# A fused attention, gated-MLP and convolution kernel: three summed attention terms for the second slot group, low parts of w_v on VectorE, a softmax split in five, and new instruction orders

## The chip, the cores and the metric

The kernel runs on one core of a Trainium2 chip. Its time is the device time in microseconds of one execution; lower is better. The time before is the median of three timed executions. The profile is of one further execution, so its own time stands beside its span.

## The reference

x is (2, 4160, 192), all data fp32. Three stages follow one another:

```python
# 1: attention over 7 taps, 8 heads of 24 channels; the weights are a softmax over the taps
w = softmax(weight_gen, axis=-1)                 # (2, 4160, 8, 7)
x = einsum('bshk,bskhg->bshg', w, unfold(x))     # row s sees rows s-6 .. s
# 2: channel mix with 1024 hidden columns
xk = mu_k * x + (1 - mu_k) * x_prev;  xr = mu_r * x + (1 - mu_r) * x_prev
k = relu(xk @ w_k);  v = (k * k) @ w_v;  y = sigmoid(xr @ w_r) * v
# 3: 1024 hidden columns, a convolution over 3 rows as a gate
h = relu(y @ w_in);  c = sum(conv_w[k] * h shifted by k - 1);  out = (h * sigmoid(c)) @ w_out
```

## The kernel before, in words

The 8320 rows of x are laid out as 128 partitions of 65 consecutive rows ("slots"). Slots are worked in 17 groups, `SIZES = [2, 4, ..., 4, 3]`; group g passes through attention, stage 2 and stage 3. The convolution of stage 3 works on window w, the same slots moved back by one, one group later. The hidden 1024 columns are 8 chunks c of 128.

Nothing is scheduled on the fly: each engine has a written order of calls (`first_steps`, then `step(i)` in a loop, then `last_steps`), and semaphores keep data right. An instruction whose data isn't there holds everything behind it on its engine. The calls that matter:

- Softmax: `softmax_front(g)` on VectorE (max, subtract), `exps(g)` on ScalarE, `softmax_back(g)` on VectorE (sum, reciprocal, product), in place in `wgt`. `SM_ENDS` splits the 66 rows of weights; a part is named by the first group that needs it: 0, 3, 7 and 11.
- Attention: `att_mult(g, k)` and `att_add(g, k)` on VectorE, 7 products and up to 6 sums. For a group in `TERMS` the taps are summed in several terms, and TensorE adds the terms up: `term_part` and the last `t_part` multiply each with the identity into PSUM (`mid`). For other groups `t_part` only transposes. `double` and `double_term` on ScalarE copy 64 channels beside themselves, for the second part.
- Mix: `z_part` (ScalarE, from PSUM), `mix_k`, `mix_r`, `mix_2` (VectorE). `x_hi`, `xr_hi_part` (ScalarE) and `x_lo`, `xr_lo_part` (VectorE) split each value into a rounded part and the rest, since fp32r products are used on TensorE: five products (`up_products`) stand for one fp32 product.
- Stage 2: `up1(g, c)`, then `k_relu`, `k_square`, `k_cast` (ScalarE), `k_lo` (VectorE), `down1(g, c)`; `r_part`, `r_sigmoid`; at the end `y_mult`, `y_hi_part`, `y_lo_part`.
- Stage 3: `up2(g, c)`, `h_relu`, `first_tap` (ScalarE), `conv_before`, `conv_after` (VectorE), `gate_sigmoid` (ScalarE), `gate` (VectorE), `down2(w, c)`, `o_copy`, and `carry`, which keeps the last slots of h.
- Weights: each is split into a rounded part and a low part. For w_k and w_v TensorE makes the low part: `low_wk`, `low_wv` add the raw weights times the identity and the rounded ones times minus the identity, `keep_wk`, `keep_wv` (ScalarE) copy it out. For w_r and w_in VectorE subtracts (`split_wr`, `split_wi`).
- `warm(n)` issues n transposes whose result nobody reads.

ScalarE uses the tables of exp and of sigmoid; each change between them is an ACT_TABLE_LOAD. DMAs of the start are issued by SP and, for the parameter rows, w_r and the first rows of the weights, by ScalarE.

The diff touches nearly every line of the written orders and these functions: the table `TERMS` (line 193), `low_wv` (408), `down1` (496), `exps` (1167), `load_wr` (1190), `keep_wv` (1207), `vals` (2238), `softmax_front` (2250), `softmax_back` (2262) and SP's list of loads (295 to 317).

Of the kernel before, what the change touches and what calls it, by code (L numbers as in the profile page):

```python
# [5 lines left out]
F32 = mybir.dt.float32  # L6
F32R = mybir.dt.float32r
ALU = mybir.AluOpType
# [6 lines left out]
def mixer_kernel(nc, x, weight_gen, mu_k, mu_r, w_k, w_v, w_r, w_in, conv_w, w_out, out):  # L15
# [58 lines left out]
    with ctx:  # L74
# [99 lines left out]
        SM_ENDS = [0, FIRST[3] + 1, FIRST[7] + 1, FIRST[11] + 1, TPP + 1]  # L174
# [18 lines left out]
        TERMS = {0: ((0, 1), (2, 3), (4,), (5, 6))}  # L193
# [89 lines left out]
        def _(sp):  # L283
# [9 lines left out]

            S0 = size(0)
# [8 lines left out]
            for n, arrived in ((1, wg2_in), (2, wg3_in)):  # L303
                lo, hi = SM_ENDS[n], SM_ENDS[n + 1] if n == 1 else TPP + 1
                sp.dma_start(wgt[:, lo * WROW:hi * WROW], wg_rows[:, (lo - 1) * WROW:(hi - 1) * WROW])\
                  .then_inc(arrived, 16)
# [5 lines left out]
            for g in range(UNIFORM + 1, 6):  # L312
                load_x(g)
            for w in range(1, NG):
                store(w)
                if w + 5 < NG:
                    load_x(w + 5)
# [27 lines left out]
        def _(pe):  # L345
# [62 lines left out]
            def low_wv(k):  # L408
                pair = slice(2 * k, 2 * k + 2)
                if k == 0:  # L410

                    pe.wait_ge(prm_ok, 1)
                if k >= 1:
                    pe.wait_ge(wv_split, 2 * k)
                low_part(od[0][:, 0:2 * D].rearrange("p (c n) -> p c n", c=2), raw_wv[:, pair, :],
                         wv_parts[:, pair, 0:D], (wv_in, 16), wv_cast, k // 2 + 1, lowv_done)

# [124 lines left out]
            def first_steps():  # L542
                term_part(0, 0, 1)
                term_part(0, 2, 1)
                term_part(0, 0, 2)
                term_part(0, 1, 1)
                term_part(0, 2, 2)
                t_part(0, 1)
                term_part(0, 1, 2)
                t_part(0, 2)  # L550
                low_wk(0)
                low_wk(1)
                low_wv(0)
# [4 lines left out]
                low_wv(1)  # L558
                up1(0, 2)
                up1(0, 3)  # L560
                r_part(0, 1)
                r_part(0, 2)
                up1(0, 4)
                warm(3)
                down1(0, 0)
                up1(0, 5)
                down1(0, 1)
                low_wv(2)
                down1(0, 2)
                t_part(1, 1)  # L570
                down1(0, 3)
                up1(0, 6)
                up1(0, 7)
                t_part(1, 2)
                low_wv(3)
# [4 lines left out]
                warm(11)  # L580
# [7 lines left out]
                r_part(1, 1)  # L588
                up2(0, 7)
                up1(1, 0)  # L590
                r_part(1, 2)
                up1(1, 1)
                up1(1, 2)
                up1(1, 3)
                up1(1, 4)
                down1(1, 0)
                up1(1, 5)
                down1(1, 1)
                up1(1, 6)
                t_part(2, 1)  # L600
                down1(1, 2)
                up1(1, 7)
                down1(1, 3)
                down1(1, 4)
                down1(1, 5)
                t_part(2, 2)
# [9 lines left out]
                up2(1, 6)  # L616
                up2(1, 7)
                r_part(2, 1)
                up1(2, 0)
                up1(2, 1)  # L620
                r_part(2, 2)
                up1(2, 2)
                down2(1, 0)
                down2(1, 1)
                up1(2, 3)
                up1(2, 4)
                down2(1, 2)
                down1(2, 0)
                up1(2, 5)
                down1(2, 1)  # L630
                up1(2, 6)
                down1(2, 2)
                up1(2, 7)
                down1(2, 3)
                down1(2, 4)
                t_part(3, 1)
                down1(2, 5)
                down1(2, 6)
                down1(2, 7)
                t_part(3, 2)  # L640
                down2(1, 3)
                down2(1, 4)
                up2(2, 0)
                up2(2, 1)
                up2(2, 2)
                up2(2, 3)
                down2(1, 5)
                up2(2, 4)
                up2(2, 5)
                down2(1, 6)  # L650
                up2(2, 6)
                up2(2, 7)
                r_part(3, 1)
                up1(3, 0)
                up1(3, 1)
                r_part(3, 2)
# [5 lines left out]
                up1(3, 5)  # L662
                down1(3, 1)
                up1(3, 6)
                down1(3, 2)
                up1(3, 7)
                down1(3, 3)
                down1(3, 4)
                down2(2, 0)
                t_part(4, 1)  # L670
                down1(3, 5)
                down1(3, 6)
                down1(3, 7)
                t_part(4, 2)
                down2(2, 1)
                down2(2, 2)
                up2(3, 0)
                up2(3, 1)
                up2(3, 2)

            def step(i):
                down2(i - 2, 3)
                up2(i - 1, 3)
                up2(i - 1, 4)
                up2(i - 1, 5)
                down2(i - 2, 4)
                up2(i - 1, 6)
                up2(i - 1, 7)
                down2(i - 2, 5)
                down2(i - 2, 6)  # L690
                r_part(i, 1)
                up1(i, 0)
                up1(i, 1)
                r_part(i, 2)
                up1(i, 2)
                down2(i - 2, 7)
                up1(i, 3)
                up1(i, 4)
                down1(i, 0)
                up1(i, 5)  # L700
                down1(i, 1)
                up1(i, 6)
                down1(i, 2)
                up1(i, 7)
                down1(i, 3)
                down1(i, 4)
                down2(i - 1, 0)
                t_part(i + 1, 1)
                down1(i, 5)
                down1(i, 6)  # L710
                down1(i, 7)
                t_part(i + 1, 2)
                down2(i - 1, 1)
                down2(i - 1, 2)
                up2(i, 0)
                up2(i, 1)
                up2(i, 2)

            def last_steps():
                down2(NG - 8, 3)  # L720
                up2(NG - 7, 3)
                up2(NG - 7, 4)
                up2(NG - 7, 5)
                down2(NG - 8, 4)
                up2(NG - 7, 6)
                up2(NG - 7, 7)
                down2(NG - 8, 5)
                down2(NG - 8, 6)
                r_part(NG - 6, 1)
                up1(NG - 6, 0)  # L730
                up1(NG - 6, 1)
                r_part(NG - 6, 2)
                up1(NG - 6, 2)
                down2(NG - 8, 7)
                up1(NG - 6, 3)
                up1(NG - 6, 4)
                down1(NG - 6, 0)
                up1(NG - 6, 5)
                down1(NG - 6, 1)
                up1(NG - 6, 6)  # L740
                down1(NG - 6, 2)
                up1(NG - 6, 7)
                down1(NG - 6, 3)
                down1(NG - 6, 4)
                down2(NG - 7, 0)
                t_part(NG - 5, 1)
                down1(NG - 6, 5)
# [2208 lines left out]
```

## Time and profile before

| | us |
|---|---|
| median of three timed executions | 717.82 |
| lowest, highest | 717.74, 718.28 |
| the profiled execution | 718.39 |
| its span, first to last instruction | 716.6 |
| TensorE busy | 706.2 (99%) |
| VectorE busy | 668.5 (93%) |
| ScalarE busy | 634.9 (89%) |
| granted TensorE clock | 1.00 over the span |

PE is TensorE, DVE VectorE, ACT ScalarE, SP SyncE; PEld is TensorE's weight load. Times are microseconds from the first instruction of the span. A matmul's duration is longer than the step from one to the next, because they overlap in the array; likewise VectorE's and ScalarE's instructions overlap their neighbours by about 0.1 us. Of a stall, the row names the engine or DMA whose event came last.

### The profile page before, as it was taken

How to read it: one execution, taken by the hardware profiler on the slowest of the kernel's cores; microseconds unless marked ns; L12 is line 12 of the kernel's file. 1: busy time of each engine (PE TensorE's matmuls, PEld its weight loads, DVE VectorE, ACT ScalarE, POOL GpSimd, SP SyncE). 2: the span in 40 equal slices, each digit the busy share in tenths (PEclk: the TensorE clock that was granted, in tenths of full speed). 3: DMA queues.
4: the chain of work that ended last, by engine and by line, in shares of the span. 5: the costliest groups of instructions: out<-in, count | busy, mean ns of one | idle time of the engine just before them, and what ended most of it. 6: DMA issues, size and time to landing. Idle time of an engine off the chain costs nothing.

```text
span 716.6 us, 10616 instructions
## 1 busy us (share of the span) xinstructions
PE 706.2 (99%) x3537; PEld 601.3 (84%) x3537; DVE 668.5 (93%) x982; ACT 634.9 (89%) x1280; POOL 3.6 (0%) x12
## 2 busy tenths in 40 slices
PE   7999999999999999999999999999999999999998
PEld 7777788888888888888887888888888888888998
DVE  6999999999999999999999999999999999987686
ACT  4998998999989899897999989998998989898975
POOL 1000000000000000000000000000000000000000
PEclk9999999999999999999999999999999999999999
DMA  9502010200202020020200102020110202000001
GB/s 257 189 27 96 1 55 1 55 23 2 78 1 77 1 77 1 1 79 0 78 1 14 65 1 78 1 78 1 26 53 1 77 1 73 1 22 1 24 1 49
DMA packets 10107, 29.86 MB, mean 42 GB/s; under 512 B 1326, under 2 KB 4936, under 8 KB 9926
## 3 DMA queue, kind: packets, MB, share of 16 engines
q1 hardware_dynamic: 9244, 28.89, 12.4%
q8 instruction: 28, 0.46, 0.3%
q10 hardware_dynamic: 810, 0.30, 0.2%
q14 instruction: 25, 0.20, 0.1%
HBM read 21.75 MB, written 6.39 MB: 39 GB/s over the span
## 4 chain that ended last, share of the span: by engine, by line
PE 81%; DVE 14%; issue 3%; ACT 2%; POOL 0%; DVEq 0%; POOLq 0%; ACTq 0%
PE up L424 34%; PE od L537 19%; PE dn L509 4%; PE dn L493 4%; PE dn L516 4%; PE dn L513 4%; PE dn L512 4%; PE dn L515 3%; DVE att L2103 2%; DVE prod L2085 2%; DVE gat L2236 2%; DVE cv L2208 2%; PE od L964 2%; PE mid L348 2%; DVE cv L2221 1%
## 5 line engine op out<-in xcount | busy, mean ns | idle before, releaser
L537 PE MATMUL od<-wo_sb,gat 128*128 128x192 f32 x1024 | 181.7, 326 | 0.1
L537 PEld LDWEIGHTS od<-wo_sb,gat 128*128 128x128 f32 x1024 | 169.9, 190 | 6.4 <-ACT o_sb L1111 0.4
L2167 DVE TENSOR_TENSOR kq_lo<-ksq,kq_hi 128x512 fp32r<-128x512 f32 (+2 forms) x136 | 90.3, 666 | 15.1 <-ACT kq_hi L1053 14.1
L1082 ACT ACTIVATE cv<-h,prm 128x512 f32<-128x512 f32 x128 | 91.7, 716 | 10.9 <-DVE gat L2236 10.3
L2208 DVE SCALAR_TENSOR_TENSOR cv<-h,prm,cv 128x512 f32<-128x512 f32 x128 | 94.9, 749 | 3.5 <-ACT cv L1082 2.4
L2221 DVE SCALAR_TENSOR_TENSOR cv<-h,prm,cv 128x512 f32<-128x512 f32 x128 | 95.6, 749 | 0.6
L2236 DVE TENSOR_TENSOR gat<-h,cv 128x512 f32<-128x512 f32 (+1 forms) x136 | 89.0, 664 | 5.2 <-ACT cv L1100 3.4
L2085 DVE TENSOR_TENSOR prod<-xin,wgt 128x768 f32<-128x768 f32 (+1 forms) x100 | 93.3, 934 | 0.0
L2103 DVE TENSOR_TENSOR att<-att,prod 128x768 f32<-128x768 f32 (+1 forms) x97 | 91.2, 941 | 0.1
L1074 ACT ACTIVATE h<-up 128x512 f32<-128x512 f32 (+2 forms) x136 | 77.4, 570 | 13.9 <-PE up L424 13.8
L1100 ACT ACTIVATE cv<-cv 128x512 f32<-128x512 f32 (+1 forms) x136 | 81.6, 605 | 5.1 <-DVE cv L2221 4.4
L1037 ACT ACTIVATE ksq<-up 128x512 f32<-128x512 f32 (+2 forms) x136 | 78.1, 579 | 7.5 <-PE up L424 4.7
L1053 ACT ACTIVATE kq_hi<-ksq 128x512 fp32r<-128x512 f32 (+2 forms) x136 | 81.7, 614 | 2.9 <-PE dn L516 1.0
L1044 ACT ACTIVATE ksq<-ksq 128x512 f32<-128x512 f32 (+2 forms) x136 | 81.6, 613 | 0.7
L424 PE MATMUL up<-y_hi,wi_hi 128*128 128x512 f32 (+2 forms) x136 | 59.2, 435 | 0.2 <-ACT h L1074 0.2
L509 PE MATMUL dn<-kq_hi,wv_parts 128*128 128x512 f32 (+2 forms) x136 | 55.3, 406 | 1.0 <-DVE kq_lo L2167 0.6
L424 PE MATMUL up<-xk_hi,wk_hi 128*128 128x512 f32 (+2 forms) x136 | 55.1, 405 | 1.0 <-ACT ksq L1037 0.9
L424 PE MATMUL up<-xk_s,wk_hi 128*128 128x512 f32 (+2 forms) x136 | 52.2, 384 | 1.2 <-DVE xk_s L2147 1.2
L424 PE MATMUL up<-y_lo,wi_hi 128*128 128x512 f32 (+2 forms) x136 | 52.5, 386 | 0.2 <-DVE y_lo L2187 0.2
L424 PE MATMUL up<-y_t,wi_lo 128*128 128x512 f32 (+2 forms) x136 | 52.6, 387 | 0.1
L424 PE MATMUL up<-y_hi,wi_lo 128*128 128x512 f32 (+2 forms) x136 | 52.4, 385 | 0.0
L516 PE MATMUL dn<-kq_lo,wv_parts 128*128 128x512 f32 (+2 forms) x136 | 52.3, 385 | 0.0
(137 smaller groups left out, 1362.2 us busy)
## 6 DMA issues: line engine op xcount, KB each, us to landing
xin<-in_x SPq DMA_DIRECT2D x14, 960.0 KB, 4.8
out<-o_sb SPq DMA_DIRECT2D x16, 384.0 KB, 3.9
wgt<-in_weight_gen SPq DMA_DIRECT2D x1, 1092.0 KB, 14.2
h<-h SPq DMA_DIRECT2D x1, 1024.0 KB, 4.5
xin<-in_x SPq DMA_DIRECT2D x1, 864.0 KB, 4.4
h<-in_moe_w_v SPq DMA_DIRECT2D x1, 768.0 KB, 10.2
wo_sb<-in_moe_w_out SPq DMA_DIRECT2D x1, 768.0 KB, 15.7
h<-in_moe_w_k SPq DMA_DIRECT2D x1, 512.0 KB, 7.1
```

What stands on the lines that cost most here:

```text
L424: mm = nc.tensor.matmul(dst[:, 0:n], w[:, cols], a[:, 0:n], start=(t == 0), stop=(t == len(terms) - 1))
L509: nc.tensor.matmul(dn[0][:, 0:n], w[:, 0:P], k_hi, start=(c == 0), stop=False)
L537: mm = nc.tensor.matmul(o, tile[:, b * P:(b + 1) * P], wo_sb[:, c, :], start=(c == 0 and b % 2 == 0), stop=(c == NC - 1), skip_group_check ...
L1044: nc.scalar.activation(ring(ksq, c, n), ring(ksq, c, n), ACT.Square).then_inc(ksq_ok, 1)
L1053: nc.scalar.activation(ring(kq_hi, c, n), ring(ksq, c, n), ACT.Copy).then_inc(kqh_ok, 1)
L1082: nc.scalar.activation(conv_tile(w, c), win(w, c, 0), ACT.Copy, scale=prm[:, 3 + NC + c:4 + NC + c])\
L2085: nc.vector.tensor_tensor(v, x, w, ALU.mult).then_inc(x_used if k == TAPS - 1 else at_mul, 1)
L2103: nc.vector.tensor_tensor(acc, acc, v, ALU.add)\
L2167: nc.vector.tensor_tensor(ring(kq_lo, c, n), ring(ksq, c, n), ring(kq_hi, c, n).bitcast(F32), ALU.subtract).then_inc(kql_ok, 1)
L2208: nc.vector.scalar_tensor_tensor(o, win(w, c, -1), prm[:, 3 + c:4 + c], base, ALU.mult, ALU.add)\
L2221: nc.vector.scalar_tensor_tensor(o, win(w, c, 1), prm[:, at:at + 1], o, ALU.mult, ALU.add)\
L2236: nc.vector.tensor_tensor(gate_tile(w, c), win(w, c, 0), conv_tile(w, c), ALU.mult).then_inc(g_ok, 1)
```

## The change

Five things are done, and the orders of all engines are written anew around them.

1. Group 1 joins `TERMS` with three terms, (0, 1), (2, 3) and (4, 5, 6): VectorE does four adds for it, not six; TensorE does four `term_part`, and its `t_part` are sums with the identity. ScalarE does `double_term(1, 0)` and `(1, 1)`.
2. The low parts of w_v are two subtractions on VectorE (`split_wv`); `low_wv` on TensorE and `keep_wv` on ScalarE are gone.
3. `SM_ENDS` has a further end: parts of 3, 8, 16, 16 and 23 rows, the second one named by group 1. `exps(0)` is followed by the copy to `minus`; the one-column sigmoid `early`, which loads the table of sigmoid, follows `exps(1)`.
4. SP loads the parameter rows and w_r; ScalarE's queue loads the two halo runs of x of the second batch. The last two loads of weight_gen become one.
5. `load_x` is issued one group later than before, the loops run to NG - 5, and `warm` calls are placed anew: after the parameter rows' transpose 1 instead of 28, then 23, 6, 4, 2, 8 and 16 instead of 3, 11 and 16.

```diff
-        SM_ENDS = [0, FIRST[3] + 1, FIRST[7] + 1, FIRST[11] + 1, TPP + 1]
+        SM_ENDS = [0, FIRST[1] + 1, FIRST[3] + 1, FIRST[7] + 1, FIRST[11] + 1, TPP + 1]
...
-        TERMS = {0: ((0, 1), (2, 3), (4,), (5, 6))}
+        TERMS = {0: ((0, 1), (2, 3), (4,), (5, 6)), 1: ((0, 1), (2, 3), (4, 5, 6))}
...
-            for a, b in HALO_RUNS:
+            for a, b in HALO_RUNS[:2]:
                 sp.dma_start(xin[a:b, 0:TAPS * D], before(x_flat, a, b, TAPS, D)).then_inc(x_in, 16)
+            for r, src in enumerate((mu_k, mu_r)):
+                sp.dma_start(prm_rows[r:r + 1, :], src[0:P].rearrange("(a n) -> a n", a=1)).then_inc(prm_in, 16)
+                sp.dma_start(prm_rows[2:3, r * D2:(r + 1) * D2], src[P:D].rearrange("(a n) -> a n", a=1))\
+                  .then_inc(prm_in, 16)
+            sp.dma_start(prm_rows[3:NPRM, :], conv_w.rearrange("k (c p) -> (k c) p", p=P)).then_inc(prm_in, 16)
+            load_wgt(SM_ENDS[1], SM_ENDS[2], wg2_in)
             load_up_weights(sp, w_k, 0, wk_in)
+            for c0, c1, at in ((0, D, 0), (P, D, D)):
+                sp.dma_start(raw_wr[:, 0, at:at + c1 - c0], w_r[0:P, c0:c1]).then_inc(wr_in, 16)
+                sp.dma_start(raw_wr[0:D2, 1, at:at + c1 - c0], w_r[P:D, c0:c1]).then_inc(wr_in, 16)
+                sp.dma_start(raw_wr[D2:P, 1, at:at + c1 - c0], w_r[P:D, c0:c1]).then_inc(wr_in, 16)
             sp.dma_start(xin[:, (TAPS + S0) * D:XSLOTS * D], x_rows[:, S0 * D:EDGE * D]).then_inc(x2_in, 16)
             sp.dma_start(raw_wv, w_v.rearrange("(c p) n -> p c n", p=P)).then_inc(wv_in, 16)
             load_up_weights(sp, w_in, 2, wi_in)
...
+            load_wgt(SM_ENDS[2], TPP + 1, wg3_in)
...
-                if eq(g, 0) and c % 2 == 0:
-                    pe.wait_ge(wv_split, c + 2)
+                if eq(g, 0) and c == 0:
+                    pe.wait_ge(wv_split, 2)
...
                 if eq(g, 0):
+                    act.wait_ge(id_ok, 2)
+                    nc.scalar.activation(minus[:, :], ident[:, :], ACT.Copy, scale=-1.0).then_inc(minus_ok, 1)
+                if eq(g, 1):
 
                     act.wait_ge(id_ok, 2)
                     nc.scalar.activation(early[:, :], ident[:, 0:1], ACT.Sigmoid).then_inc(early_ok, 1)
-                    load_wr()
-                    nc.scalar.activation(minus[:, :], ident[:, :], ACT.Copy, scale=-1.0).then_inc(minus_ok, 1)
...
+            for a, b in HALO_RUNS[2:]:
+                act.dma_start(xin[a:b, 0:TAPS * D], before(x_flat, a, b, TAPS, D)).then_inc(x_in, 16)
...
+            def split_wv():
+                dve.wait_ge(wv_cast, 2)
+                nc.vector.tensor_tensor(wv_parts[:, :, 2 * P:3 * P], raw_wv[:, :, 0:P],
+                                        wv_parts[:, :, 0:P].bitcast(F32), ALU.subtract).then_inc(wv_split, 1)
+                nc.vector.tensor_tensor(wv_parts[:, :, D:2 * P], raw_wv[:, :, P:D],
+                                        wv_parts[:, :, P:D].bitcast(F32), ALU.subtract).then_inc(wv_split, 1)
```

ScalarE's order of the start, new (one line stands for the calls in this order):

```
exps(0); double_term(0,1), (0,2), (0,0); exps(1); cast_wk(); double(0); z_part(0,0), (0,1); cast_wr(); x_hi(0,1);
z_part(0,2); xr_hi_part(0,1); keep_wk(0), (1); x_hi(0,2); keep_wk(2); xr_hi_part(0,2); z_carry(0); cast_wi(0); ...
```

VectorE's order of the start, new:

```
softmax_front(0); softmax_back(0); att_mult(0,0), (0,1); att_add(0,1); att_mult(0,2), (0,3), (0,4); att_add(0,3);
softmax_front(1); att_mult(0,5), (0,6); params(); att_add(0,6); softmax_back(1); mix_k(0); mix_r(0); att_mult(1,0);
x_lo(0,1); mix_2(0); att_mult(1,1); x_lo(0,2); att_add(1,1); split_wr(); xr_lo_part(0,1); att_mult(1,2), (1,3);
xr_lo_part(0,2); att_add(1,3); att_mult(1,4), (1,5); k_lo(0,0); att_mult(1,6); split_wv(); att_add(1,5); k_lo(0,1);
att_add(1,6); k_lo(0,2), (0,3); split_wi(0); k_lo(0,4); split_wi(1); mix_r(1); mix_k(1); k_lo(0,5), (0,6);
att_mult(2,0); k_lo(0,7); att_mult(2,1); y_mult(0,1), (0,2); y_lo_part(0,1), (0,2); mix_2(1); x_lo(1,1); ...
```

TensorE's order of a steady step, new. Before, `down2(w, 0)` to `(w, 2)` stood between `down1(g, 4)` and `up2(g, 0)`, the other five among up2 and the next up1:

```
up1(g,5); down2(w,0); down1(g,1), (g,2); up1(g,6); down1(g,3); up1(g,7); down1(g,4); down2(w,1); t_part(g+1,1);
down2(w,2); t_part(g+1,2); down1(g,5) .. (g,7); down2(w,3) .. (w,5); up2(g,0) .. (g,7); r_part(g+1,1), (g+1,2);
up1(g+1,0) .. (g+1,2); down2(w,6); up1(g+1,3); down2(w,7); up1(g+1,4); down1(g+1,0)         with w = g - 1
```

The later softmax parts on VectorE. Before: front(7) after `k_lo(1,5)`, back(7) after `att_mult(5,3)`; front(11) after `conv_before(7,1)`, back(11) after `conv_after(8,3)`. New: front(7) after `gate(3,1)` and back(7) after `gate(4,4)`; front(11) after `gate(7,1)`, back(11) after `gate(8,4)`, which in both cases is followed by one more gate, mix_r and y_mult. `exps(3)` on ScalarE stood after `h_relu(0,6)` and stands after `k_cast(1,3)`.

## Rows read from the trace of the kernel before

**Rows 1.** From the page: busy time by engine; the chain that ended last, by engine.

```profile
PE 706.2 (99%) x3537; PEld 601.3 (84%) x3537; DVE 668.5 (93%) x982; ACT 634.9 (89%) x1280; POOL 3.6 (0%) x12
...
PE 81%; DVE 14%; issue 3%; ACT 2%; POOL 0%; DVEq 0%; POOLq 0%; ACTq 0%
```

**Rows 2.** Busy by stretch: stretch, length, busy (instructions) per engine, clock, DMA share, GB/s.

```profile
231.19:272.67 41.48, 41.48 (x205) 35.26 (x203) 39.31 (x57) 37.17 (x74) 0.00 (x0) 1.00 0.10 34
...
314.15:399.61 85.46, 84.39 (x406) 69.87 (x406) 84.89 (x119) 77.69 (x151) 0.00 (x0) 1.00 0.11 33
```

**Rows 3.** The chain in order of time: start, us, engine, tile, line, count.

```profile
4.05 6.40 PE od L964 x30
...
13.83 4.04 PE mid L355 x36
...
51.50 1.28 ACT L1063
...
71.37 1.75 PE od L964 x16
...
141.89 1.30 PE od L537 x8
...
183.78 1.30 PE od L537 x8
...
225.53 1.30 PE od L537 x8
...
325.92 1.42 DVE smx L2259
327.36 1.50 DVE wgt L2260
...
378.29 1.42 DVE smx L2270
...
381.35 1.50 DVE wgt L2273
```

**Rows 4.** Timeline of VectorE, the start: start, us, line, operation, shapes, [idle before <- releaser].

```profile
4.24 0.80 DVE L2259 TENSOR_REDUCE smx<-wgt 128x88 f32<-128x616 f32 x1 [3.34 <-DMA wgt<-in_weight_gen]
...
9.37 0.76 DVE L2085 TENSOR_TENSOR gat<-xin,wgt 128x576 f32<-128x576 f32 x1
...
15.51 0.76 DVE L2103 TENSOR_TENSOR att<-att,prod 128x576 f32<-128x576 f32 x1
...
19.04 0.48 DVE L2135 SCALAR_TENSOR_TENSOR xr<-mid,prm,zr 128x256 f32<-128x256 f32 x1 [1.81 <-ACT zr L988]
```

**Rows 5.** Timeline of VectorE at y_mult(0,1) and x_lo(1,1).

```profile
41.56 0.43 DVE L2177 TENSOR_TENSOR y<-dn,y 128x256 f32<-128x256 f32 x1
...
42.24 0.68 DVE L2144 TENSOR_TENSOR xk_lo<-xk,xk_hi 128x512 fp32r<-128x512 f32 x1
```

**Rows 6.** Timeline of SP: the four loads of x's halo rows.

```profile
1.64 1.77 SPq L298 DMA_DIRECT2D xin<-in_x  x4
```

**Rows 7.** DMA issues: count, KB each, median us from issue to landing.

```profile
xin<-in_x SPq DMA_DIRECT2D x2, 252.0 KB, 5.2
```

**Rows 8.** Timeline of ScalarE in the start.

```profile
6.64 1.28 ACT L1178 ACT_TABLE_LOAD   x1
...
7.93 0.20 ACT L1178 ACTIVATE early<-ident 128x1 f32<-128x1 f32 x1
...
14.72 1.04 ACT L1199 ACTIVATE wk_hi<-h 128x1024 fp32r<-128x1024 f32 x1
...
18.43 0.57 ACT L988 ACTIVATE zr<-mid,omu 128x384 f32<-128x384 f32 x1
```

**Rows 9.** Timeline of TensorE around low_wv(1).

```profile
26.83 0.81 PE L398 MATMUL od<-h,ident 128*128 128x384 f32 x2
...
27.65 0.28 PE L424 MATMUL up<-xk_hi,wk_hi 128*128 128x256 f32 x1
```

**Rows 10.** Timeline of VectorE at y_mult(1,1).

```profile
71.48 0.69 DVE L2177 TENSOR_TENSOR y<-dn,y 128x512 f32<-128x512 f32 x1 [0.66 <-PE dn L516]
```

More of the change, by code:

```diff
@@ L969, in _ @@
             nc.tensor.transpose(od[0][:, 0:NPRM], prm_rows[:, :], ident[0:NPRM, 0:NPRM]).then_inc(prm_t, 1)
-            warm(28)
+            warm(1)
             first_steps()
-            for i in range(4, NG - 6):
+            for i in range(4, NG - 5):
                 step(i)
@@ L1381, in first_steps @@
+                k_square(2, 1)
+                k_relu(2, 2)
+                k_cast(2, 1)
+                r_sigmoid(2, 2)
+                k_relu(2, 3)
+                k_square(2, 2)
+                k_cast(2, 2)
+                k_square(2, 3)
+                gate_sigmoid(1, 2)
+                k_cast(2, 3)
+                k_relu(2, 4)
+                k_relu(2, 5)
+                k_square(2, 4)
+                gate_sigmoid(1, 3)
                 k_cast(2, 4)
                 k_square(2, 5)
+                first_tap(1, 5)
@@ L1499, in first_steps @@
+                k_relu(4, 1)
+                k_cast(4, 0)
+                k_square(4, 1)
                 gate_sigmoid(3, 2)
+                k_relu(4, 2)
+                k_cast(4, 1)
+                r_sigmoid(4, 2)
+                k_relu(4, 3)
+                k_square(4, 2)
+                o_copy(2, 0)
+                o_copy(2, 1)
+                k_cast(4, 2)
+                k_square(4, 3)
                 exps(7)
-                first_tap(3, 4)
-                r_sigmoid(4, 1)
+                k_cast(4, 3)
@@ new lines, in step @@
+                k_square(i + 1, 5)
+                first_tap(i, 6)
+                k_cast(i + 1, 5)
+                k_relu(i + 1, 6)
+                first_tap(i, 7)
+                k_square(i + 1, 6)
+                carry(i, 1)
+                k_cast(i + 1, 6)
+                k_relu(i + 1, 7)
+                double(i + 2)
+                k_square(i + 1, 7)
+                gate_sigmoid(i, 4)
+                k_cast(i + 1, 7)
+                gate_sigmoid(i, 5)
+                carry(i, 2)
@@ L1741, in last_steps @@
-                z_carry(NG - 4)
-                k_square(NG - 4, 3)
-                k_relu(NG - 4, 4)
+                k_relu(NG - 4, 2)
+                k_cast(NG - 4, 1)
+                r_sigmoid(NG - 4, 2)
+                k_relu(NG - 4, 3)
+                k_square(NG - 4, 2)
+                o_copy(NG - 6, 0)
+                o_copy(NG - 6, 1)
+                k_cast(NG - 4, 2)
+                k_square(NG - 4, 3)
+                k_cast(NG - 4, 3)
+                k_relu(NG - 4, 4)
+                k_relu(NG - 4, 5)
@@ L1888, in last_steps @@
+                k_cast(NG - 2, 1)
+                r_sigmoid(NG - 2, 2)
+                k_relu(NG - 2, 3)
+                k_square(NG - 2, 2)
+                o_copy(NG - 4, 0)
+                o_copy(NG - 4, 1)
+                k_cast(NG - 2, 2)
+                k_square(NG - 2, 3)
+                k_cast(NG - 2, 3)
+                k_relu(NG - 2, 4)
+                k_relu(NG - 2, 5)
+                first_tap(NG - 3, 5)
+                double(NG - 1)
+                k_square(NG - 2, 4)
                 gate_sigmoid(NG - 3, 3)
-                o_copy(NG - 4, 0)
@@ L2032, in _ @@
             first_steps()
-            for i in range(4, NG - 6):
+            for i in range(4, NG - 5):
                 step(i)
@@ L2755, in last_steps @@
             def last_steps():
+                x_lo(NG - 3, 2)
+                gate(NG - 4, 0)
+                att_add(NG - 2, 2)
+                conv_after(NG - 4, 1)
+                att_mult(NG - 2, 3)
+                conv_after(NG - 4, 2)
+                conv_before(NG - 4, 3)
+                att_mult(NG - 2, 4)
+                att_add(NG - 2, 3)
+                k_lo(NG - 3, 0)
+                gate(NG - 4, 1)
+                conv_after(NG - 4, 3)
                 conv_before(NG - 4, 4)
+                att_mult(NG - 2, 5)
@@ L2929, in _ @@
             first_steps()
-            for i in range(4, NG - 6):
+            for i in range(4, NG - 5):
                 step(i)
```

1916 lines of the change are left out of this document (829 added, 1087 removed).

## The prediction

> **What bounds the kernel now.** I read the page first: TensorE is busy 99% of the span and carries 81% of the chain that ended last, VectorE 14% [rows 1]. So I look for the places where TensorE does something other than needed work. The second view, busy time by stretch, answers for the middle. One group of four slots takes 41.48 us with TensorE busy in all of it and VectorE in 39.31; the stretch from 314.15 to 399.61 us holds two groups and takes 85.46 us instead of 82.96 [rows 2]. 2.5 us are lost there, and VectorE, busy 84.89 of 85.46, has no slack in it. In the chain in order of time one and the same down2 piece stands at 141.89, 183.78 and 225.53 us: periods of 41.89 and 41.75, 0.4 and 0.3 over. The 2.5 us lie around the softmax of the last 23 rows (front at 325.92, back at 378.29) [rows 3], the 0.7 us around the back part of the 16 rows before them. The third view, the timeline, is for the start: the first term part runs on TensorE at 13.83 [rows 3]; VectorE starts attention of slot group 0 at 9.37, its last add at 15.51, then waits 1.81 us for zr and mixes at 19.04 [rows 4]. From there to y_mult of group 0 at 41.56 [rows 5] it is nearly solid. So up to about 41 us VectorE sets the pace, with warm transposes on TensorE; after that TensorE does.
>
> **Part by part.**
>
> *First softmax part of 3 rows, not 11.* VectorE's passes fall from 616 to 168 elements. A pass of 616 took 0.80 us [rows 4], one of 1288 took 1.50 [rows 3]: 1.04 ns an element, so 168 cost 0.35. Reduce, subtract, exp, reduce, add, reciprocal and product come to some 2.5 us instead of the 5.1 from 4.24 to 9.33: ready at 6.7. Now the halo rows of x bind. Their last load was issued at about 3.0 [rows 6] and the larger ones land in 5.2 [rows 7], so at 8.2; with 224 KB less in front (0.9 us at the page's 257 GB/s) at 7.4, bounds 6.6 and 9.4. Attention of group 0 starts 1.9 us sooner.
>
> That lead is handed back before it reaches anything. Its nine steps are 0.68 each (from 9.37 to 15.51). Between them stands front(1), eight rows, 1.3 us, and params, 0.3: the last add begins at 7.4 + 6.1 + 1.6 = 15.1 against 15.51. On ScalarE exps(1) can't start before front(1) ends, 7.4 + 7 x 0.68 + 1.3 = 13.5. Behind it are queued exp 0.6, the load of the sigmoid table 1.29 and `early` 0.2, two casts of w_k of 0.95, double(0) 0.25 and two z parts of 0.5 [rows 8], a step being 0.1 less than a duration. The sum puts zr at 18.8 and the first mix at 18.9 against 19.04. The table load was hidden before (at 6.64, beside the softmax); its cover is gone. TensorE's own queue allows little more: 30 transposes end at 10.45 [rows 3], then a term of 0.67 (4.04 for six of them), warm(23) at 0.11 and four terms: t_part(0,1) at 16.5, so z at 17.4 at the earliest.
>
> The Trainium skill, page "ScalarE: Activation LUTs", section "What ACT_TABLE_LOAD costs", has a switch of tables cost the 1.28 us load and a drain of 1.38 more. Here the load at 6.64 is followed by the next activation at 7.93: 1.29 us and no drain [rows 8], and the measurement decides. By the page's 2.66 the start would come 1.4 us later and the whole change be worth 0.6 instead of 2.0.
>
> *From the mix to y_mult(0), on VectorE.* Added: split_wr, 0.7, which lay in the wait for zr before; split_wv, two passes of 1024 and 512 elements, 1.21 and 0.68 by the pass of 512 (0.68, [rows 5]) and 1.04 ns an element, as steps 1.74 (bounds 1.5 and 2.0). Gone: two att_adds of group 1, 768 elements, 0.87 each, 1.74. Net +0.7, less 0.1 for the earlier mix: y_mult(0) at about 42.1, 0.5 later. But x_lo(1,1), at 42.24 between y_mult and y_lo [rows 5], moves behind y_lo, and up2(0,0) needs y_lo in its third product: 0.5 comes back. I take 0 for up2(0,1), at 44.0; bounds -1.2 (table load hidden, x at 6.6) and +1.5 (x at 9.4, or ScalarE slips).
>
> *TensorE in the start.* low_wv goes: 26.83 to 27.65 is 0.82 [rows 9], four are 3.3 us. Term parts of group 1 are 4 x 8 matmuls at 0.112 (4.04 over 36, [rows 3]), 3.6 us; t_part(1) becomes 16 of them for 8 transposes, +0.9. Net +1.2 us, hidden by the waits for xr_lo, split_wv (down1(0,0) at 32.4 by the sum above) and k_lo; uncovered it costs 1.2. ScalarE loses the eight copies of keep_wv (about 2.1 us as steps) and gains two doubles (0.6). SP issues five parameter loads and six of w_r ahead of x2, w_v and w_in; the bytes in front of w_in are what they were, so it lands where it did. load_x(w + 4) now stands behind store(w), which waits for the copy of the last down2 of window w; its x is used some 20 us later by the order of the steps and takes 5 to land, so nothing. The parameters, now behind halo rows in one queue, must be there when the transposes end at 10.45; I expect 7.5 to 8.5, so nothing is paid.
>
> *Group 1.* exps(3) brings two table loads; the chain runs through the one at 51.50 [rows 3], in front of r_sigmoid and k_relu. In the new order it stands behind k_cast(1,3), with no sigmoid until the gates; front(7), 2 us of VectorE, leaves the stretch before y_mult(1). The warm(16) at 71.37 stays [rows 3]. I take -0.5, bounds -1.1 and +0.5.
>
> *Steady groups.* The same work in another order. down2 3, 4 and 5 (three of 1.30, [rows 3]) now fill the time between down1(7) and up2(0), where two pieces did. y_mult waits 0.66 for the last down1 [rows 10], and y_mult, y_hi, y_lo need 2.4 us before they stop up2, so y_mult may now be 1.5 us late unnoticed. I take 41.48 a period again: 0; bounds -0.2 and +1.2 (0.1 in each of twelve).
>
> *Softmax of the last rows.* VectorE's slack is 41.48 - 39.31 = 2.17 a group [rows 2]. Front(11) is 2.94 (325.92 to 328.86), back(11) 4.56 (378.29 to 382.85) [rows 3]. Both fall between y_mult(7) and y_mult(9), two groups: 7.5 - 4.3 - 1.5 = 1.7 us lost, against 2.5. Front(7) and back(7) are 0.7 of that by elements, 5.3: less than 5.8, nothing lost, against 0.7. The fronts stand before k_lo(·,1), which my walk through the new orders has 3.7 us ahead of its down1 (an estimate from steps of 0.6 to 0.87 on VectorE and the period above), so they are absorbed in place. Sum -1.5; bounds -3.2 (all of it gone) and +1.6 (rival 2).
>
> *The tail* I leave at 0, within 0.3.
>
> Sum: 0 - 0.5 + 0 - 1.5 + 0 = -2.0 us. The profiled execution took 718.39 us for a span of 716.6; the median of the three timed is 717.82. So span 714.6, profiled execution 716.4, median 715.8.
>
> **Rivals.**
>
> 1. More: the start does gain. If the table load doesn't hold the z parts, the mix moves to 17.9, and if softmax loses nothing: -1.1 - 0.5 - 3.2 = -4.8, 713.0. For it: VectorE idles 0.9 us at 18 in my walk. Against: the load stands in the queue, and z can't precede 17.4.
>
> 2. Slower: back(7) and back(11) stand just ahead of y_mult, the one chain that has little beside it. If VectorE's 2.17 us are spent at other waits, back delays y_mult in full: 3.2 - 1.5 and 4.6 - 1.5 make 4.8 lost against 3.2, and with group 1's gain gone it is +1.6: 719.4. It decides from y_mult 3 us late. For it: only 0.66 of the slack sat at y_mult. Against: the other waits were on ScalarE, which the new order moves too.
>
> 3. Nothing: start +0.5, the 1.2 us of TensorE half uncovered, a softmax that loses 2.1: 717.8.
>
> 4. A late start: x or the parameters land after 10.5, +2.2 at the first mix; with -1.0 later 719.0.
>
> **Chances.** Forecast 0.45 (a fifth of it within 0.2%; own range 714.4 to 717.0), rival 1 0.17, rival 3 0.19, rival 2 0.14, rival 4 0.05. What a measurement of this kernel can tell from no change is 0.2%, 1.4 us. Faster 0.36 + 0.17 = 0.53, same 0.09 + 0.19 = 0.28, slower 0.14 + 0.05 = 0.19. The range of 712.8 to 719.2 goes from rival 1 to short of rival 2.
>
> **What would show it.** att_mult(0,0) at 7.4; a table load on ScalarE at 14.1 and the first mix at 18.9; y_mult(0) at 42.1; up2(0,1) at 44.0 as before; y_mult(1) at 71.0 for 71.48; periods of 41.48; the two groups around both parts of the last softmax at 84.7 together; no mark of back(7). It is wrong if up2(0,1) moves by over 1.5 us, if a steady period is not 41.48, or if y_mult after back(11) comes over 3 us late.

## The result, and the profile after

The changed kernel takes 721.82 us (median of four executions, 721.35 to 723.41) against 717.78 before; the ratio is 1.0058, interval 1.0046 to 1.0069. It is 4.0 us slower, where 2.0 us faster was forecast. Its profiled execution took 721.35 us with a span of 719.6, 3.0 more than the span of before.

From the page of the changed kernel, the busy time by engine and the chain that ended last by engine, to be read against [rows 1]:

```profile
PE 707.5 (98%) x3567; PEld 602.3 (84%) x3567; DVE 667.1 (93%) x988; ACT 633.5 (88%) x1275; POOL 3.6 (0%) x12
...
PE 82%; DVE 11%; ACT 3%; issue 2%; DMA 1%; ACTq 0%; DVEq 0%
```

TensorE has 1.3 us more work in a span 3.0 us longer: most of the loss is idle time. Where it is, the stretches from one up2(g,0) to another show, in the columns of [rows 2]: a steady group, the two groups around the last softmax part, and then the three groups behind them.

```profile
237.59:279.15 41.56, 41.56 (x204) 35.15 (x204) 39.76 (x58) 38.05 (x77) 0.00 (x0) 1.00 0.10 34
320.67:404.55 83.88, 83.73 (x407) 70.17 (x406) 83.31 (x116) 75.46 (x148) 0.00 (x0) 1.00 0.10 34
404.55:449.40 44.85, 42.28 (x205) 34.83 (x203) 41.12 (x60) 41.22 (x87) 0.00 (x0) 1.00 0.09 32
449.40:492.00 42.60, 42.02 (x204) 34.96 (x203) 41.02 (x65) 37.18 (x75) 0.00 (x0) 1.00 0.10 33
492.00:533.56 41.56, 41.56 (x204) 35.15 (x204) 38.94 (x57) 37.02 (x75) 0.00 (x0) 1.00 0.10 34
```

The softmax of the last rows costs less than before, as forecast: 83.88 us for two groups. But group 10, which took 41.49 us before, takes 44.85 with TensorE busy in only 42.28 of them, and group 11 takes 42.60. The timeline of ScalarE in group 10 has the place, and that of TensorE the consequence:

```profile
418.00 0.73 ACT L1050 ACTIVATE cv<-h,prm 128x512 f32<-128x512 f32 x1 [0.53 <-DVE gat L2116]
418.63 2.43 ACT L1058 ACTIVATE wgt<-h,prm 128x128 f32<-128x128 f32 x8
420.97 0.40 ACT L1124 ACTIVATE h<-h 128x256 f32<-128x256 f32 x1
421.27 0.57 ACT L1005 ACTIVATE ksq<-up 128x512 f32<-128x512 f32 x1
```

```profile
419.34 0.40 PE L425 MATMUL up<-xk_s,wk_lo 128*128 128x512 f32 x1
421.90 0.51 PE L425 MATMUL up<-xk_hi,wk_hi 128*128 128x512 f32 x1 [2.17 <-ACT ksq L1005]
```

The eight activations at 418.63 are `early_center`, which prepares the convolution across the seam of the two batches. `if i == 8` puts all of them behind the last call of one single step, in both kernels. But a step is not the same stretch in both: the steps are cut anew, and the 8 now names a place one group earlier. In the kernel before, the block on ScalarE ran in group 11 and its partner on VectorE in group 12; in the changed kernel they run in groups 10 and 11, closer behind the last softmax part. From the timelines of ScalarE and VectorE before:

```profile
453.75 2.44 ACT L1090 ACTIVATE wgt<-h,prm 128x128 f32<-128x128 f32 x8
...
506.87 2.19 DVE L2227 SCALAR_TENSOR_TENSOR wgt<-h,prm,wgt 128x128 f32<-128x128 f32 x8
```

In the new order of ScalarE that place is in front of carry(9,0) and k_relu(10,0); up1(10,2) needs the bank that k_relu(10,0) empties, and TensorE stands still for 2.17 us. One group later its partner on VectorE, `early_after`, does the same on a smaller scale in front of a piece of x_lo(11,2), and group 11 takes 1.1 us more than a steady one:

```profile
459.24 2.18 DVE L2107 SCALAR_TENSOR_TENSOR wgt<-h,prm,wgt 128x128 f32<-128x128 f32 x8
461.45 0.69 DVE L2027 TENSOR_TENSOR xk_s<-xkr,xk_s 64x512 fp32r<-64x512 f32 x1
```

The prediction did not mention these calls. The start went as its walk had it. From the timelines of VectorE and ScalarE:

```profile
7.65 0.76 DVE L1965 TENSOR_TENSOR gat<-xin,wgt 128x576 f32<-128x576 f32 x1 [1.28 <-DMA xin<-in_x]
...
18.98 0.48 DVE L1995 SCALAR_TENSOR_TENSOR xk<-mid,prm,zk 128x256 f32<-128x256 f32 x1 [0.94 <-ACT zr L956]
...
42.32 0.43 DVE L2057 TENSOR_TENSOR y<-dn,y 128x256 f32<-128x256 f32 x1 [0.15 <-PE dn L517]
...
71.58 0.69 DVE L2057 TENSOR_TENSOR y<-dn,y 128x512 f32<-128x512 f32 x1 [0.55 <-PE dn L517]
```

```profile
14.37 1.28 ACT L1149 ACT_TABLE_LOAD   x1
15.66 0.20 ACT L1149 ACTIVATE early<-ident 128x1 f32<-128x1 f32 x1
```

Attention begins at 7.65 (forecast 7.4), the table load stands at 14.37 (14.1), the mix at 18.98 (18.9), y_mult(0) at 42.32 (42.1). The y_mult of group 1 stands at 71.58, 0.1 later than in [rows 10] where 0.5 earlier was forecast.

### The profile page after: what moved, and what is told of

The parts are those of the page before. It is cut to its first block, busy times and chain, and to the rows that moved or that the text cites. A ratio compares the mean times of both kernels' runs of the same rounds, so it can differ in the third digit from the quotient of the medians.

```text
span 719.6 us, 10666 instructions
## 1 busy us (share of the span) xinstructions
PE 707.5 (98%) x3567; PEld 602.3 (84%) x3567; DVE 667.1 (93%) x988; ACT 633.5 (88%) x1275; POOL 3.6 (0%) x12
## 4 chain that ended last, share of the span: by engine, by line
PE 82%; DVE 11%; ACT 3%; issue 2%; DMA 1%; ACTq 0%; DVEq 0%
PE up L425 35%; PE od L538 21%; PE dn L510 4%; PE dn L494 4%; PE dn L517 4%; PE dn L513 4%; PE dn L514 4%; PE dn L516 3%; DVE prod L1965 2%; PE mid L359 2%; DVE cv L2088 1%; DVE gat L2116 1%; DVE att L1983 1%; DMA xin<-in_x 1%; DVE kq_lo L2047 1%
## 5 line engine op out<-in xcount | busy, mean ns | idle before, releaser
L1965 DVE TENSOR_TENSOR prod<-xin,wgt 128x768 f32<-128x768 f32 (+1 forms) x98 | 91.1, 931 | 0.1
L1983 DVE TENSOR_TENSOR att<-att,prod 128x768 f32<-128x768 f32 (+1 forms) x93 | 87.1, 937 | 0.3
L425 PE MATMUL up<-xk_hi,wk_hi 128*128 128x512 f32 (+2 forms) x136 | 56.8, 418 | 2.9 <-ACT ksq L1005 2.9
L425 PE MATMUL up<-y_hi,wi_hi 128*128 128x512 f32 (+2 forms) x136 | 56.2, 414 | 0.6 <-ACT y_hi L993 0.3
L425 PE MATMUL up<-xk_s,wk_lo 128*128 128x512 f32 (+2 forms) x136 | 52.3, 385 | 0.0
L425 PE MATMUL up<-xk_lo,wk_hi 128*128 128x512 f32 (+2 forms) x136 | 52.3, 384 | 0.0
```

The costliest lines, as they stand in the source:

```text
L425: mm = nc.tensor.matmul(dst[:, 0:n], w[:, cols], a[:, 0:n], start=(t == 0), stop=(t == len(terms) - 1))
L1965: nc.vector.tensor_tensor(v, x, w, ALU.mult).then_inc(x_used if k == TAPS - 1 else at_mul, 1)
L1983: nc.vector.tensor_tensor(acc, acc, v, ALU.add)\
```

## The experiments

In each, up2(g,0) is the first product of up2 of group g. "Period g" is the time from up2(g-1,0) to up2(g,0), numbered by the group that it ends with; the group called 10 above is period 10. In the changed kernel three more pieces of down2 stand ahead of up2(g,0) from group 3 on, so positions of the two orders are compared only by the periods or at the end. The median of before was taken anew beside the runs (717.86 to 717.97 us); each ratio is to the one taken beside it.

### The once-only calls of step 8

**e1_center_moved.** The changed kernel with early_center behind x_hi(i+2,2). In the order of before it stands behind the same call, but of the next group, x_hi(11,2):

```diff
                 x_hi(i + 2, 2)
+                if i == 8:
+                    for c in range(NC):
+                        early_center(c)
...
-                if i == 8:
-                    for c in range(NC):
-                        early_center(c)
```

> The changed kernel, with the eight early_center activations of ScalarE (2.43 us, once, in step 8) moved from the end of the step, in front of carry(9,0) and k_relu(10,0), to behind x_hi(10,2), where the kernel before has them. Theory A: standing there they held back k_relu(10,0), and so up1(10,2), by 2.3 us; moved, that is gone: 719.5, and TensorE's gap at 422 us is below 0.3. Rival B: group 10 is late because VectorE and ScalarE arrive there without slack, whatever stands in front; the 2.3 us turn up elsewhere and the time stays 721.8 within 0.4.

720.76 us, ratio to before 1.0039 (1.0024 to 1.0053). Period 10 goes from 44.85 to 44.11 and the idle time of TensorE moves to 420.81 and shrinks from 2.17 to 1.06 us:

```profile
420.81 0.50 PE L425 MATMUL up<-xk_hi,wk_hi 128*128 128x512 f32 x1 [1.06 <-ACT ksq L1005]
```

Neither expectation held: the stop moved and halved with the block, which ties it to the block, but most of the time stayed. So the neighbour of before gives little relief here, one group earlier. How much the block costs in all, the next run shows.

**e2_early_late.** The changed kernel with both blocks taken out of step 8, and one call at a time in `last_steps`:

```diff
                 carry(NG - 3, 0)
+                early_center(0)
...
                 conv_after(NG - 2, 0)
+                early_after(0)
```

> The changed kernel, with early_center and early_after taken out of step 8 and spread one by one over the last steps, behind carry(14, c) on ScalarE and conv_after(15, c) on VectorE, where both engines have slack. Theory A: the periods of 44.85 and 42.61 us fall to 41.6 each, 3.3 + 1.0 less: 717.6 to 718.2. Rival B: under 1.5 less, over 720.3. If early_center alone is the cause, 719.4.

718.95 us, 1.0015 (1.0005 to 1.0024): 2.9 us of the loss gone, but 0.75 us above the upper end of what theory A expected. The periods 10 to 12:

```profile
404.80:447.30 42.50, 42.08 (x204) 34.83 (x203) 40.85 (x60) 39.12 (x79) 0.00 (x0) 1.00 0.10 33
447.30:488.82 41.52, 41.52 (x204) 35.12 (x204) 38.93 (x57) 36.97 (x75) 0.00 (x0) 1.00 0.10 34
488.82:530.40 41.58, 41.58 (x204) 35.11 (x204) 38.91 (x57) 36.99 (x75) 0.00 (x0) 1.00 0.10 34
```

From up2(9,0) to up2(12,0) it takes 125.60 us, against 129.01 in the changed kernel: 3.4 us. About 1 us of it is given back in the last three groups, where TensorE's timeline has two short waits that the changed kernel doesn't have, 0.18 us each, at 657.71 and 684.87; they show only a part of it. What is left in period 10 (42.50) shows mostly as the y chain behind the softmax: TensorE waits 0.34 us for y_lo at 405.84. The run moved both blocks. That the one on ScalarE made period 10 late and the one on VectorE period 11 rests on the timelines, and on e1, in which only the first was moved and period 11 stayed at 42.64.

**b2_early_late_only.** The same edit in the kernel before.

> The kernel before with one edit: early_center and early_after one by one in the last steps (behind carry of window 14 and conv_after of window 15), not at the end of step 8. Theory (in the order of before they cost only the 0.27 us by which the period of group 12, 41.74, is over 41.47): 717.65 us. Rival (they fill idle time there, and in the last steps they are late): 718.2 us or more.

717.56 us, 0.9997 (0.9988 to 1.0007). Period 12 falls from 41.74 to 41.47 and no wait appears in the tail. The same two blocks cost 0.27 us in the old order and 3.4 in the new one, one group earlier. No run has them one step later in the new order (`i == 9`). The trace of the changed kernel lets one estimate what that would save: in its groups without the block k_relu(g,0) ends 0.31 to 0.38 us before up1(g,2) starts (groups 3 to 9), and ScalarE mostly idles 0.2 us in front of it. That is room for about 0.5 us of the block's 2.3, so by this estimate most of the cost is the new place's and not the group's. This is the fastest version of the study, by less than the measurement can tell.

### Start or rest

**h_new_start, h_old_start.** Each takes one kernel's orders of all engines up to a seam in group 0 (warm(8) or warm(11) on TensorE, y_hi_part(0,3) on ScalarE, mix_2(1) and x_lo(1,1) on VectorE), and the other's from there:

```
h_new_start:  after ... warm(8)   | before: up2(0, 0) ...
h_old_start:  before ... warm(11) | after:  up2(0, 0) ...
```

> All of the change up to y_lo_part(0, 2), so the three terms, split_wv, the softmax part of three rows and the loads by SP, and behind it the orders of the kernel before, from up2(0,0) and h_relu(0,0) on. It tells what the named parts of the change are worth without the new orders. Theory A (they are worth nothing): up2(0,1) 0.4 us later than before, then the old orders: 718.2, between 717.6 and 718.8. Rival C, the start causes the loss (a later backlog on VectorE): 720 or more. Rival D, the start gains and only the orders lose: 716.5 or less.

> The other half: the kernel before up to mix_2(1), and behind it the orders of the changed kernel from up2(0,0) on. None of the three terms for group 1, split_wv, the small softmax part or the moved loads. Theory A: the loss is in the orders behind the start, so it is all here: 721.0 to 722.0. Rival C: 718 or less.

With the new start alone 718.93 us, 1.0014 (1.0005 to 1.0023); with the rest alone 722.25 us, 1.0058 (1.0043 to 1.0073). So the rest holds most of the loss. The sum of the two, 5.3 us, is more than the 4.0 of the whole, for the reason that the stretches of h_old_start around its stop at 421.10 show:

```profile
404.00:418.00 14.00, 13.59 (x57) 10.25 (x57) 13.81 (x21) 13.36 (x29) 0.00 (x0) 1.00 0.00 0
418.00:424.00 6.00, 3.81 (x14) 3.02 (x14) 5.45 (x8) 6.00 (x16) 0.00 (x0) 0.84 0.00 0
424.00:430.00 6.00, 6.00 (x28) 5.28 (x27) 4.68 (x7) 4.62 (x10) 0.00 (x0) 0.87 0.06 23
```

The column before the last two is the granted clock. TensorE had idled 2.19 us; 1.4 us after it came back it stepped as at the lower of its two levels (a matmul of 192 columns every 0.32 us instead of 0.16), for some 3 us; shares of 0.84 and 0.87 of the full clock mean that it was at 1.2 GHz in a part of each stretch. Period 10 takes 46.53 us there, against 44.85 in the profiled execution of the changed kernel, which idled as long and kept its clock. All four executions of h_old_start have a mean clock of 0.998, of the changed kernel only the one of 723.41 us.

### The parts of the start, one at a time

All four are made from the kernel before. One caution comes first, from comparing that kernel with b2_early_late_only, whose start is the same. The chain of b2_early_late_only begins so:

```profile
4.04 5.40 PE od L964 x30
...
12.83 4.41 PE mid L355 x36
```

In [rows 3] the same 30 transposes take 6.40 us, and the first product of the term parts comes at 13.83. The transposes step at 0.21 us at first and at 0.11 later, the lower and the upper of TensorE's two levels by that factor of two (the granted clock reads 1.00 over both). The change of pace came between 6.9 and 9.9 us in the thirteen other profiled executions and at 10.07 in that of before, so its whole start is 0.65 late: up2(1,0) at 72.98, against 72.33 in b2_early_late_only, 72.30 in b3_late_and_new_place and 72.25 in h_old_start, which have the same start. The starts below are compared with 72.33.

**s_wv_on_vector.** Only the low parts of w_v on VectorE:

```diff
-                low_wv(0)
...
-                keep_wv(0)
...
                 att_mult(1, 5)
+                split_wv()
```

> The kernel before with one part of the change: the low parts of w_v by split_wv on VectorE (behind att_mult(1,5)), low_wv and keep_wv gone. Theory (VectorE sets the pace of the start up to y_mult of group 0): 1.74 us more on VectorE put up2(0,0) from 42.59 to 44.3 us, and 1.2 to 1.7 of it stay to the end, 719.4 us. Rival (TensorE and ScalarE pace it as much, and lose 3.3 and 2.1 us of work): up2(0,0) within 0.5 us of 42.59, 717.9 us.

719.53 us, 1.0022 (1.0013 to 1.0032); up2(1,0) at 73.99, 1.66 later. The 1.74 us of VectorE are paid nearly in full, and the 3.3 us of TensorE saved bring nothing.

**s_three_terms.** Only the three terms of group 1:

```diff
-        TERMS = {0: ((0, 1), (2, 3), (4,), (5, 6))}
+        TERMS = {0: ((0, 1), (2, 3), (4,), (5, 6)), 1: ((0, 1), (2, 3), (4, 5, 6))}
```

> The kernel before with another part of the change alone: group 1 in three terms that TensorE sums (four term parts more and sums for transposes, 4.5 us of TensorE; two att_add less, 1.74 us of VectorE; two doubles more on ScalarE). Theory (VectorE sets the pace): up2(0,0) from 42.59 to 41.2 us, 716.6 us. Rival (TensorE has no room of 4.5 us there, with low_wv still in its queue): up2(0,0) at 42.6 or later, 718 us or more.

721.20 us, 1.0043 (1.0028 to 1.0058); up2(1,0) at 75.25, 2.9 later. VectorE's work falls, and the time goes up. The busy times from 26 us to where up2(0,0) stood before, in the columns of [rows 2], first of the kernel before, then with the terms:

```profile
26.00:42.60 16.60, 15.97 (x119) 14.46 (x119) 16.42 (x28) 15.35 (x45) 0.00 (x0) 1.00 0.18 62
```

```profile
26.00:42.60 16.60, 16.60 (x134) 15.81 (x133) 12.36 (x21) 12.99 (x42) 0.00 (x0) 1.00 0.19 62
```

Before, both engines were nearly full: TensorE 15.97 and VectorE 16.42 of 16.60. With the terms TensorE is busy in all of it and VectorE in 12.36. Of TensorE's time before, about 0.6 us was idle and 0.3 the three transposes of warm(3), which the terms replace; the 4.5 us of work that come leave 3.6 to be paid by this reckoning, and 2.9 were.

**s_terms_and_wv.** Both.

> The kernel before with three terms for group 1 and the low parts of w_v on VectorE, both. Alone they put up2(0,0) 2.5 and 1.0 us later. Theory (TensorE is full between 26 and 42 us with the terms, VectorE with split_wv; each part frees what the other fills): up2(0,0) 0.6 to 1.2 us later than 42.59, 718.9 us. Rival (the two costs add up): 3.5 us later, 721.5 us.

720.43 us, 1.0038 (1.0023 to 1.0053); up2(1,0) at 74.58, 2.25 later: less than the 4.6 of the sum, and less than the terms alone, so each part does make room for the other; but more than the 0.6 to 1.2 expected. The excess fits the clock. TensorE idles 2.01 us up to 25.32, and in the stretch behind it the granted clock is 0.64:

```profile
25.30:30.00 4.70, 4.68 (x27) 4.70 (x28) 4.67 (x6) 3.36 (x10) 0.00 (x0) 0.64 0.02 8
```

A full clock would have done the same in 4.70 x 0.64 = 3.0 us; without the 1.7 us, if all of them reach the end of the start, this profile would be 0.6 later than the start of before; no execution of this kernel kept the clock (0.998 in all four). In s_wv_on_vector TensorE idles as long at the same place (2.02 us) and keeps 1.00 in the profile; three of its ten executions have 0.998, and their median is 720.0 us against 719.4 of the other seven. There a fall cost 0.6 us, so the 1.7 is the most that it can be here.

**s_small_softmax.** Only the first softmax part of three rows (with the sigmoid behind exps(1)):

```diff
-        SM_ENDS = [0, FIRST[3] + 1, FIRST[7] + 1, FIRST[11] + 1, TPP + 1]
+        SM_ENDS = [0, FIRST[1] + 1, FIRST[3] + 1, FIRST[7] + 1, FIRST[11] + 1, TPP + 1]
```

> The kernel before with one part of the change: softmax parts of 3 and 8 rows in place of 11, exps(1) with the sigmoid behind it in front of the casts of w_k, softmax_front(1) behind att_add(0,3), softmax_back(1) behind params. Theory (the table load hands the lead back): first product near 7.6 instead of 9.37, but the first mix at 18.9 to 19.4 instead of 19.04, up2(0,0) within 0.3 us of 42.6, 718.0 us. Rival (part of the lead gets through): the first mix before 18.3, 717.2 us.

719.42 us, 1.0021 (1.0012 to 1.0031); up2(1,0) at 74.08. Attention begins at 8.08 instead of 9.37, but the first mix comes at 20.15, later than both expectations. ScalarE holds it:

```profile
14.67 1.28 ACT L1184 ACT_TABLE_LOAD   x1
15.97 0.20 ACT L1184 ACTIVATE early<-ident 128x1 f32<-128x1 f32 x1
16.08 1.04 ACT L1202 ACTIVATE wk_hi<-h 128x1024 fp32r<-128x1024 f32 x1
17.02 1.04 ACT L1203 ACTIVATE wk_hi<-h 128x1024 fp32r<-128x1024 f32 x1
...
19.55 0.57 ACT L990 ACTIVATE zr<-mid,omu 128x384 f32<-128x384 f32 x1
```

**s_no_early_table.** h_new_start without the one-column sigmoid, so that its table is loaded when r_sigmoid(0,1) first needs it:

```diff
-                if eq(g, 1):
-                    act.wait_ge(id_ok, 2)
-                    nc.scalar.activation(early[:, :], ident[:, 0:1], ACT.Sigmoid).then_inc(early_ok, 1)
```

> The kernel h_new_start (new start, then the orders of before; 718.93 us, up2(0,0) at 43.49) without the one-column sigmoid behind exps(1), so that the table of sigmoid is loaded only at r_sigmoid(0,1), near 29 us. Theory (the load of 1.28 us holds the z parts): zr ends at 17.8 instead of 19.0, the first mix is at 17.9 to 18.1 instead of 19.06, up2(0,0) at 42.6, 718.0 us. Rival (TensorE paces the start as well, and the load only moves to the casts of k): the mix comes 1 us earlier but up2(0,0) stays at 43.2 or later, 718.7 us or more.

719.88 us, 1.0031 (1.0019 to 1.0043), 1.0 us slower than h_new_start, not faster. The mix does come at 18.42 instead of 19.06, but nothing of that arrives; the load, now at 29.26, delays the casts of k behind it, and up2(1,0) stands at 74.41 instead of 73.52.

### The softmax of the last rows

**e3_softmax_old_place.** e2 with the two calls where the order of before had them:

```diff
                 x_lo(i + 3, 1)
+                if i == 5:
+                    softmax_front(11)
...
                 conv_after(i + 1, 3)
+                if i == 7:
+                    softmax_back(11)
```

> The changed kernel with the early carry work in the last steps (718.95 us in its own run), and here softmax_front(11) and softmax_back(11) back at the places that they had before: the front behind conv_before(7,1), the back behind conv_after(8,3). Theory (the places brought the gain of the softmax): the two periods around it, 42.31 and 41.60 in that run, become 42.1 and 43.4 as before, 1.6 us more, 720.5 us. Rival (the new order as a whole has more room for the softmax, wherever it stands): both periods together stay under 84.2, 719.0 us.

721.78 us, 1.0052 (1.0037 to 1.0067). Periods 8 to 10 take 129.18 us, against 126.41 in e2: the places are worth 2.8 us in the new order. The front part now holds up xk_s, for which TensorE waits 1.05 us at 334.27, and the back part a k_lo:

```profile
389.83 0.50 PE L510 MATMUL dn<-kq_hi,wv_parts 128*128 128x512 f32 x1 [1.46 <-DVE kq_lo L2052]
```

**b3_late_and_new_place.** b2 with the two calls at the places of the changed kernel, behind gate(7,1) and gate(8,4).

> The kernel before with two edits: early_center and early_after one by one in the last steps, and softmax_front(11) behind gate(7,1), softmax_back(11) behind gate(8,4), as in the changed kernel. Theory (places): the two periods around the softmax, 42.10 and 43.37, lose 1.6 together, and the period of group 12 (41.74) loses 0.3: 716.0 us. Rival (the gain needs the new order): back(11) stands two calls ahead of y_mult in the order of before and delays it, the two periods stay at 85.4 or more, and only 0.3 is gained: 717.6 us or more.

720.85 us, 1.0035 (1.0023 to 1.0048). Periods 8 to 10 take 130.53 us, before 126.96: 3.6 more. Not all of it is the places: behind the wait shown below the granted clock is 0.87 (402 to 405 us) and 0.73 (405 to 410), by the reckoning above 0.4 and 1.35 us, 1.7 in all. So by estimate the places cost 1.9 us in the old order and the clock that fell behind the wait the rest. The two executions of six with a mean clock of 1.000 agree: 719.83 and 720.16 us, 2.3 and 2.6 over b2. First VectorE, then TensorE:

```profile
398.83 1.50 DVE L2278 TENSOR_TENSOR wgt<-wgt,smx 128x1288 f32<-128x1288 f32 x1
400.25 0.74 DVE L2120 SCALAR_TENSOR_TENSOR xk<-mid,prm,zk 128x512 f32<-128x512 f32 x1
400.91 0.68 DVE L2182 TENSOR_TENSOR y<-dn,y 128x512 f32<-128x512 f32 x1
```

```profile
402.40 0.47 PE L424 MATMUL up<-y_hi,wi_hi 128*128 128x512 f32 x1 [2.38 <-ACT y_hi L1025]
```

This is the mechanism of rival 2: back(11) just ahead of y_mult delays it. In the order of before it does; in the new order, which has three pieces of down2 in front of up2(g,0) instead of two among other changes, waits of some 0.7 us are left behind it.

## Why the prediction was wrong

**The step that failed** is "Steady groups. The same work in another order", taken at 0 with bounds of -0.2 and +1.2. It priced the calls that repeat in every group and left out the two blocks that run once, in step 8, although they are in the written order, 2.43 us on ScalarE and 2.18 on VectorE, and although the same `i == 8` puts them one group earlier than before. They cost 3.4 us in the changed kernel (2.9 at the end) and 0.3 before. The slack of a whole group would not have shown it, since ScalarE has 41.48 - 37.17 = 4.3 us of it [rows 2]: the two orders could, by what the block stands in front of and what waits for that call. The steady periods themselves are 41.53 on average instead of 41.48, some 0.05 us in each of ten, without a wait that the trace names.

**The start and group 1**, forecast at 0 and -0.5. In the two profiles up2(1,0) moved by +0.1, but [rows 3] came from an execution with a late start. Against the same start in another execution it is +0.75, and the median of h_new_start says +1.0. Four of the walk's moments were met within 0.3 us and up2(0,1) within 0.5 (44.44 for 44.0), and still the conclusion was wrong, since it was compared with a first mix at 19.04 and an up2(0,0) at 42.59 that stand at 18.41 and 41.98 in b2_early_late_only. By size this is the second step that failed: 0.75 to 1.0 us lost where 0.5 was to be gained. The view "up to about 41 us VectorE sets the pace" was half right: s_wv_on_vector shows that VectorE has no slack there, and s_three_terms that TensorE has next to none either (15.97 of 16.60 us busy, three transposes of warm(3) among them). The net 1.2 us of TensorE that I hid behind waits had little to hide behind. The parts alone, in the old order of the start, put up2(1,0) 1.66, 2.9 and 1.75 us later, together in the new order 0.75 in the changed kernel and 1.2 in the profile of h_new_start; which of the moved calls wins that back was not tried. The gain of 0.5 in group 1 did not come; y_mult(1) waits for down1, thus for TensorE.

**The table load** held the z parts, as forecast, and rival 1's hope did not come true: with the load out of the way the mix comes 0.6 us earlier, at 18.42 and not at 17.9, and the kernel gets slower, since the load then holds other calls. The switch from exp to sigmoid takes 14.37 to 15.66 in the changed kernel, 1.29 us. The Trainium skill, page "ScalarE: Activation LUTs", section "What ACT_TABLE_LOAD costs", adds a drain of 1.38 us to a switch; no row here has it, as in [rows 8].

**The softmax parts** gave what was forecast: the 16 rows lose 0.1 instead of 0.7 us, periods 8 to 10 lose 1.8 (in e2_early_late, 126.41 us against three of 41.55) in place of 2.5 (126.96 against three of 41.48), in all 1.3 of the 1.5. The argument for it, that fewer elements or more slack in sum decide, is not what decides: e3 and b3 put the same instructions elsewhere by a few calls and lose 2.8 and about 1.9 us more (3.6 with the fall of the clock). Rival 2 was right about the mechanism and wrong about where it applies.

**The size.** The sum by what was measured: start +0.75 to +1.0, softmax -1.3, blocks +3.1, ramp of groups 2 and 3 +0.5, pace +0.5, tail -0.1. That is 3.5 to 3.7 us of the 4.0, and the rest is open. The clock hardly has a part in it: one of the four executions has a mean clock of 0.998 (723.41 us), and the median of the other three is 721.76. That the trace shows 3.0 where the medians show 4.0 comes from the late start of the profile before (0.65) for the greater part.

**Still open** are the 0.5 us of the ramp (one gap of 0.29 us in TensorE's steps, at 83.45, is all that shows) and the 0.05 of the pace, in the start what SP's loads contribute, which were not tried alone, and how much of the 3.4 us would be left with the blocks one group later.

## What to carry to other kernels

When a written order is replaced, find the calls that run once (`if i == 8`) first, look which group the number names in the new steps, and price them: a block of 2.4 us is harmless or costs nearly its whole length, by what stands behind it, and it is cheap to cut it in pieces and move these to where nothing waits. A cost or gain measured for a placement belongs to that order alone; the same places of the softmax calls are worth 2.8 us in one order and cost about 1.9 in the other, and 1.1 more (between the medians) in the executions in which the clock falls behind the wait. And before a walk is compared with a trace to a few tenths, look at how far two executions of the same start differ.

## What the runs showed of the hardware

TensorE's pace in the first transposes, 0.21 us a step and then 0.11, changes at a moment that differs between executions by 3 us (6.86 to 10.07 us in 14 profiles) though TensorE began to work at 4.04 to 4.06 in all of them; in the profile of the kernel before, where it came at 10.07, up2(1,0) stood 0.65 us later than in three profiles of the same start in which it came at 7.9 to 9.2. An idle time of 2.0 to 2.4 us may be followed by a stretch at the lower level: the granted clock was 0.84 and 0.87 in h_old_start, 0.64 in s_terms_and_wv and 0.87 and 0.73 in b3_late_and_new_place (402 to 405 and 405 to 410 us), and stayed at 1.00 after 2.17 us in the changed kernel and after 2.02 and 2.12 in s_wv_on_vector. By the mean clock of each execution (0.998 for 1.000) it fell in one of four of the changed kernel, in four of four of h_old_start and of s_terms_and_wv, in four of six of b3_late_and_new_place and in three of ten of s_wv_on_vector. Between the medians of the executions with and without it the fall cost 1.65 us in the changed kernel, 1.1 in b3 and 0.6 in s_wv_on_vector. What decides is not shown.
